# Local-and-summary attention and two MLPs: softmax kept in the PSUM bank of its scores, three units normalised by one instruction

## The reference, cut to what matters

```python
scores_l = scale * q @ k.T                       # masked to |i - j| < 16
scores_s = scale * q @ k_sum.T + log(32)         # k_sum: max over blocks of 32 keys
scores_all = concat([where(mask_l, scores_l, -1e9), scores_s])
a = exp(scores_all - max(scores_all))
a = a / (sum(a) + 1e-9)
x = a @ concat([v, v_sum])                       # v_sum: mean over blocks of 32 values
...
h = x @ w_in;  g = max(h, 0) + alpha * min(h, 0);  x = g @ w_out        # first MLP, 2048 wide
h = x @ w_in2; g = P(h) / (Q(h) + 1e-6);          out = g @ w_out2      # second MLP, rational activation
```

## Time and profile before

| | us |
|---|---|
| median of 3 runs | 654.24 |
| lowest and highest | 653.11 and 656.0 |
| span of the profiled execution, first to last instruction | 652.5 |
| PE busy | 619.4 (95%) |
| DVE busy | 487.2 (75%) |
| ACT busy | 345.9 (53%) |
| POOL busy | 208.5 (32%) |

### The profile page before, as it was taken

The page is one execution under the profiler, slowest core; times in us unless marked ns, Lnnn a source line. Parts: engine busy times, 40 slices in busy tenths (PEclk is TensorE's granted clock), DMA queues, the critical chain, the costliest instruction groups (busy, mean ns, idle before and its releaser), DMA issues.

```text
span 652.5 us, 9963 instructions
## 1 busy us (share of the span) xinstructions
PE 619.4 (95%) x3504; PEld 586.2 (90%) x3504; DVE 487.2 (75%) x1056; ACT 345.9 (53%) x838; POOL 208.5 (32%) x217
## 2 busy tenths in 40 slices
PE   5777899999999999999999997899999999999997
PEld 4767899999999999999999996899999999999995
DVE  3877767555666556555555589999999999999995
ACT  4686544343343353342333275666765576567654
POOL 4545984000000000000122356455443334444431
PEclk9898989999999999999999999999999999999999
DMA  8879920221022201200344410000100010001001
GB/s 183 191 186 244 260 59 14 60 60 41 21 60 48 48 17 33 48 1 4 94 130 130 129 33 1 1 2 0 49 1 1 2 49 0 2 1 49 1 1 49
DMA packets 82211, 37.56 MB, mean 58 GB/s; under 512 B 59761, under 2 KB 76145, under 8 KB 81777
## 3 DMA queue, kind: packets, MB, share of 16 engines
q1 hardware_dynamic: 82160, 36.92, 22.2%
HBM read 32.58 MB, written 3.15 MB: 55 GB/s over the span
## 4 chain that ended last, share of the span: by engine, by line
PE 82%; DVE 11%; ACT 2%; issue 1%; ACTq 0%; DVEq 0%
PE acc L852 12%; PE acc L854 12%; PE acc L853 12%; PE hid L852 9%; PE hid L854 9%; PE hid L853 9%; PE att L852 3%; PE att L854 3%; PE att L853 3%; PE att L841 3%; DVE probs L677 2%; PE att L820 2%; PE att L788 1%; PE att L827 1%; DVE poly L767 1%; DVE g_lo L739 1%
## 5 line engine op out<-in xcount | busy, mean ns | idle before, releaser
L852 PE MATMUL hid<-x_hi,w_in_hi 128*128 128x384 f32 x384 | 130.5, 340 | 0.6 <-DVE x_lo L684 0.6
L854 PE MATMUL hid<-x_hi,w_in_lo 128*128 128x384 f32 x384 | 129.6, 338 | 0.0
L853 PE MATMUL hid<-x_lo,w_in_hi 128*128 128x384 f32 x384 | 129.4, 337 | 0.0
L428 POOL TENSOR_TENSOR w_out_lo<-w_out_raw,w_out_hi 128x512 fp32r<-128x512 f32 x32 | 42.8, 1337 | 246.8 <-ACT w_out_hi L456 246.8
L446 POOL TENSOR_SCALAR qpart<-habs,ab 128x384 f32<-128x384 f32 x64 | 52.3, 817 | 137.8 <-ACT poly L601 136.6
L852 PE MATMUL acc<-g_hi,w_out_hi 128*128 128x384 f32 x256 | 90.9, 355 | 0.0
L853 PE MATMUL acc<-g_lo,w_out_hi 128*128 128x384 f32 x256 | 87.0, 340 | 0.0
L854 PE MATMUL acc<-g_hi,w_out_lo 128*128 128x384 f32 x256 | 87.0, 340 | 0.0
L700 DVE TENSOR_TENSOR g_lo<-g_full,g_hi 128x384 fp32r<-128x384 f32 x64 | 41.2, 644 | 55.3 <-ACT g_hi L456 55.1
L852 PE MATMUL acc<-w_out_hi,g_hi 128*128 128x512 f32 x192 | 76.1, 396 | 5.7 <-DVE g_lo L739 5.7
L854 PE MATMUL acc<-w_out_hi,g_lo 128*128 128x512 f32 x192 | 76.1, 396 | 0.0
(11 more groups left out here) (119 smaller groups left out, 1262.0 us busy)
## 6 DMA issues: line engine op xcount, KB each, us to landing
w_in_raw<-in_moe_w_in_dram SPq DMA_DIRECT2D x32, 256.0 KB, 4.1
w_out_raw<-in_moe_w_out_dram SPq DMA_DIRECT2D x16, 512.0 KB, 4.1
vw<-in_v_dram SPq DMA_DIRECT2D x32, 120.0 KB, 2.6
q_raw<-in_q_dram SPq DMA_DIRECT2D x32, 96.0 KB, 2.6
vs_raw<-in_v_dram SPq DMA_DIRECT2D x4, 768.0 KB, 7.4
out_dram<-out_sb SPq DMA_DIRECT2D x12, 256.0 KB, 2.0
k_raw<-in_k_dram SPq DMA_DIRECT2D x16, 104.0 KB
k_raw<-in_k_dram SPq DMA_DIRECT2D x16, 100.0 KB
```

Source lines behind the costliest of these rows:

```text
L428: pool.tensor_tensor(w_out_lo[:, f, :], w_out_raw[:, f, :], w_out_hi[f][:, :].bitcast(F32), ALU.subtract).then_inc(pool_w_out, 1)
L852: pe.matmul(dst, lhs[0], rhs[0], start=start, stop=False)
L853: pe.matmul(dst, lhs[0], rhs[1], start=False, stop=False)
L854: return pe.matmul(dst, lhs[1], rhs[0], start=False, stop=stop)
```

## The change

The scores stay in the PSUM bank in which PE made them. DVE's masking instruction writes them back to the same columns of `bk[g]`, ACT's exponential works there in place, and its row sums go to three columns at the end of the same bank (columns 384 to 386). `psums` in SBUF goes. `pden` is computed from those columns. The normalisation of a group is one `tensor_tensor` in place of three `tensor_scalar`: it multiplies the 3 x 120 exponentials in PSUM by the three reciprocals, broadcast along the columns from SBUF, and writes `probs` in SBUF. PE's transposes read `probs` as before. No wait is added, removed or moved; the number of ACT and PE instructions stays.

```diff
+        def scores_of(bk, g, u):
+            u -= g * GU
+            return bk[g][:, u * KU:(u + 1) * KU]
+
+        def sums_of(bk, g):
+
+            return bk[g][:, GU * P:GU * P + GU]
...
-                            last = act.activation(probs[:, s, u, :], probs[:, s, u, :], ACT.Exp, scale=-1.0,
-                                                  bias=nmax[:, s, u:u + 1], accum_out=psums[:, s, u:u + 1])
+                            last = act.activation(scores_of(bk, g, u), scores_of(bk, g, u), ACT.Exp, scale=-1.0,
+                                                  bias=nmax[:, s, u:u + 1], accum_out=sums_of(bk, g)[:, u - g * GU:u - g * GU + 1])
...
-                            last = dve.tensor_tensor_reduce(probs[:, s, u, :], bk[g][:, (u - g * GU) * KU:(u - g * GU + 1) * KU],
+                            last = dve.tensor_tensor_reduce(scores_of(bk, g, u), scores_of(bk, g, u),
                                                             mask[:, unit_mask(j, u), :], -1.0 / SQRT_D, 3.0e38,
                                                             ALU.add, ALU.min, nmax[:, s, u:u + 1])
...
-                        dve.tensor_scalar(pden[:, s, us], psums[:, s, us], 1.0e-9, None, ALU.add).then_inc(dve_den, 1)
+                        dve.tensor_scalar(pden[:, s, us], sums_of(bk, g), 1.0e-9, None, ALU.add).then_inc(dve_den, 1)
...
-                        for u in range(g * GU, (g + 1) * GU):
-                            last = dve.tensor_scalar(probs[:, s, u, :], probs[:, s, u, :], prec[:, s, u:u + 1], None, ALU.mult)
-                        last.then_inc(dve_p, 1)
+                        dve.tensor_tensor(probs[:, s, us, :], bk[g][:, 0:GU * KU].rearrange("p (u k) -> p u k", u=GU),
+                                          prec[:, s, us].unsqueeze(2).broadcast_to([P, GU, KU]), ALU.mult).then_inc(dve_p, 1)
```

More of the change, by code:

```diff
@@ L129, in attention_two_mlps @@
     nmax = place("nmax", [P, 2, UNITS])
-    psums = place("psums", [P, 2, UNITS])
     pden = place("pden", [P, 2, UNITS])
```

## The result

| | before | changed kernel |
|---|---|---|
| median, us | 653.67 | 648.54 |
| lowest and highest, us | 652.9 to 656.0 | 648.21 to 649.69 |
| ratio to before, 95% interval | 1 | 0.9908 [0.9886, 0.993] |
| span of the profiled execution, us | 652.5 | 646.4 |

The forecast was 647.0 us with a range of 643 to 651. The changed kernel is 0.9% faster than the one before by the recorded ratio (0.8% by the two medians), and 1.5 us short of the forecast. The forecast took 7.2 us off a median of 654.24. Against the 653.67 us measured beside it the changed kernel gains 5.1 us, and its profiled span is 6.1 us shorter. Its profiled execution took 648.21 us for a span of 646.4, so the distance between the two is 1.8 us, where the forecast had 1.7.

The account below looks back on a forecast made before the run. PE is fully busy from 115 to 300 us; only its earlier stalls, with DVE held by POOL, can go. 0.3 + 4.0 + 1.6 + 1.3 = 7.2 us off 654.24 gives 647.0 us, range 643 to 651.

Parts of the forecast that it names:

- fifth term: From TR of job 6 to the end of the span: forecast 0 us, since everything there shifts as a whole.
- What is held, and by what: Ahead of 115 us: POOL holds DVE instructions with all sources in SBUF, by up to 1.1 us each.
- broadcast operand in SBUF is held all the same: Normalisation: the broadcast reciprocals make the multiplication wait for POOL, one hold a group; 4.2 us gained, 650.0 us, chance 0.13.
- The multiplication: Normalisation of a group: one instruction of 529 ns in place of three taking 0.67 us, 0.14 us shorter undisturbed.
- `pden`, masking, exponentials: Attention chain: `pden` 169 ns undisturbed, masking change taken as 0 within 0.1 us, six exponentials together 0.2 us shorter.
- PSUM instructions are late in every job: Jobs 7 to 15: over 0.08 us more per instruction stalls PE; 661 us at 0.25 us each, chance 0.05.
- Step 4, the landing: Job 5's queries: they land at 65.7 us and hold PE, idle about 3.8 us, limiting the gain to 1.9 us.
- this landing does not move: Job 5's queries: nothing ahead of their issue in SP's queue waits for the attention, so they land at 65.7 us.
- Step 4, the clock: Behind PE's wait for job 5's queries: the clock falls once more, costing 1.6 us.
- no fall of the clock: Behind the DMA wait for job 5's queries: clock stays up; 8.8 us less, 645.4 us, chance 0.15.
- Step 6 and step 10: TR of job 5 gains 4.0 us, the clock behind it 1.6, TR of job 6 1.3; POOL's wait isn't reached.
- What comes later shifts as a whole: After TR of job 6: PE is never idle to 300 us, so the rest moves earlier unchanged.

## Experiments: what held DVE

The theory is that an instruction of DVE is held by POOL when all its sources are in SBUF. Its rival is that fewer instructions do it, wherever their sources are. A further doubt was whether POOL is what holds them. Four kernels part these. The first keeps PSUM and gives back the three instructions:

```diff
-                        dve.tensor_tensor(probs[:, s, us, :], bk[g][:, 0:GU * KU].rearrange("p (u k) -> p u k", u=GU),
-                                          prec[:, s, us].unsqueeze(2).broadcast_to([P, GU, KU]), ALU.mult).then_inc(dve_p, 1)
+                        for u in range(g * GU, (g + 1) * GU):
+                            last = dve.tensor_scalar(probs[:, s, u, :], scores_of(bk, g, u), prec[:, s, u:u + 1], None, ALU.mult)
+                        last.then_inc(dve_p, 1)
```

> The changed kernel with the normalisation of a group cut back into three tensor_scalar instructions, each reading its 120 exponentials from PSUM. If the gain comes from where the source lies (theory): each multiplication stays at 0.25 to 0.32 us with POOL busy, none is held, TR of jobs 5 and 6 has no idle time, and the time is that of the changed kernel, 648.5 us, up to 1 us more. If it comes from one instruction in place of three, so that DVE meets POOL less often (rival): multiplications of up to 1.3 us are back, with 2 to 4 us of idle time of PE in TR of jobs 4 to 6, and the time is 651 to 653 us.

It took 647.25 us, ratio 0.9906 [0.9884, 0.9928], the time of the changed kernel within the intervals (the expectation had 648.5 and up). The line view of 10 to 115 us, where POOL works, has 24 of the 42 instructions in this row; the 18 in the other banks are at 334 to 344 ns:

```profile
L684 DVE TENSOR_SCALAR probs<-att,prec x24: 332/334/344, 14.2 to 95.9; 128x120 f32<-128x120 f32 x24
```

None is held. Each takes 334 ns, though, where the same instruction took 276 ns from SBUF: from PSUM it is 58 ns longer, and above the 0.25 to 0.32 us that was expected. PE still waits 0.77 and 0.62 us in TR of job 4, so a short wait there is no sign of a hold. In TR of jobs 5 and 6 it doesn't wait.

The second is the kernel before with the one instruction, and both sources in SBUF:

```diff
-                        for u in range(g * GU, (g + 1) * GU):
-                            last = dve.tensor_scalar(probs[:, s, u, :], probs[:, s, u, :], prec[:, s, u:u + 1], None, ALU.mult)
-                        last.then_inc(dve_p, 1)
+                        dve.tensor_tensor(probs[:, s, us, :], probs[:, s, us, :],
+                                          prec[:, s, us].unsqueeze(2).broadcast_to([P, GU, KU]), ALU.mult).then_inc(dve_p, 1)
```

> The kernel before, its scores, exponentials and sums in SBUF, with only the three multiplications of a group made one tensor_tensor, both sources in SBUF. Theory (the place of the source): the one instruction is held by POOL and ranges from 0.53 to 1.7 us, pden from 0.15 to 1.3 us, PE is idle for 0.5 to 2 us in TR of job 5; 650 to 652 us. Rival (fewer instructions are what counts): it stays under 0.8 us nearly always and the time is 648 to 649.5 us, that of the changed kernel.

It took 647.39 us, ratio 0.9902 [0.9882, 0.9922]. The lines in 10 to 115 us, then PE's timeline at TR of jobs 4 and 5:

```profile
L676 DVE TENSOR_TENSOR probs<-probs,prec x14: 532/533/1462, 14.1 to 99.6; 128x360 f32<-128x360 f32 x14
...
L672 DVE TENSOR_SCALAR pden<-psums x14: 157/170/2055, 13.7 to 99.2; 128x3 f32<-128x3 f32 x14
```

```profile
55.14 0.85 PE L826 MATMUL att<-ident,probs 128*120 128x128 f32 x3 [2.21 <-DVE probs L676]
...
80.25 0.54 PE L826 MATMUL att<-ident,probs 128*120 128x128 f32 x3 [2.19 <-DVE probs L676]
```

Here DVE is held as before, up to 1462 and 2055 ns, but once for the multiplication of a group in place of up to three times. PE still stands 2.2 us in TR of job 4 and of job 5, and not at all in TR of job 6. At 647.39 us both expected ranges were missed (650 to 652 and 648 to 649.5). The kernel is as fast as the changed one by its median and not by the same way. PE comes to job 5's keys late enough (65.78 us) not to wait for the DMA, so it loses no clock there, and it doesn't have the loss of the fifth term (its period of four steps, explained below, is 20.73 us). So equal times say nothing here on the theory; the rows do. They show that the source decides on the hold, and the number of instructions on how often it is paid.

The third is the changed kernel with the row sums back in SBUF, so that `pden` alone reads SBUF. `psums` is again where it was:

```diff
+    psums = place("psums", [P, 2, UNITS])
...
-                                                  bias=nmax[:, s, u:u + 1], accum_out=sums_of(bk, g)[:, u - g * GU:u - g * GU + 1])
+                                                  bias=nmax[:, s, u:u + 1], accum_out=psums[:, s, u:u + 1])
...
-                        dve.tensor_scalar(pden[:, s, us], sums_of(bk, g), 1.0e-9, None, ALU.add).then_inc(dve_den, 1)
+                        dve.tensor_scalar(pden[:, s, us], psums[:, s, us], 1.0e-9, None, ALU.add).then_inc(dve_den, 1)
```

> The changed kernel with the row sums back in SBUF (psums), so that pden has its source in SBUF and is the only instruction of the chain that POOL can hold. Theory: pden ranges from 0.15 to 1.3 us while POOL splits weights and stays at 0.17 us without POOL; job 5's chain has about 0.9 us to spare in the changed kernel, so at most one such hold is covered and PE is idle for 0 to 1.5 us in TR of jobs 5 and 6; 648.5 to 650.5 us. Rival (the part of pden is nothing): 648.5 us and no idle time.

Groups by line (busy us, mean ns of one) in 10 to 115 us, and PE's timeline at TR of job 4:

```profile
L680 DVE TENSOR_SCALAR pden<-psums 128x3 f32<-128x3 f32 x14 | 6.7, 482 | 1.9 <-ACT att L496 1.0 <-ACT acc L496 0.6
...
L684 DVE TENSOR_TENSOR probs<-att,prec 128x360 f32<-128x360 f32 x8 | 4.3, 533 | 0.3
```

```profile
51.70 0.54 PE L834 MATMUL att<-ident,probs 128*120 128x128 f32 x3 [0.47 <-DVE probs L684]
53.34 0.55 PE L834 MATMUL att<-ident,probs 128*120 128x128 f32 x3 [1.10 <-DVE probs L684]
```

The multiplication is free at 533 ns and `pden`, three columns, is held to 482 ns on average. That costs 1.57 us ahead of TR of job 4, where PE would have waited for the DMA anyway, and nothing in job 5. The time is 644.95 us, ratio 0.9861 [0.9842, 0.9881]: faster than the changed kernel by 3.6 us of medians, and under the 648.5 us from which both expectations started, although it does strictly worse on DVE. Of the 3.4 us between the two profiled spans, 1.6 lie behind TR of job 6: this was the first sign that the place of the tiles matters. Another 1.2 us lie behind job 5's queries, where the clock did not fall in this execution (11.12 us to TR of job 5 for 12.32).

The fourth leaves DVE as it was before and takes POOL's work away (what it leaves out is said in its expectation):

```diff
-                pool.tensor_tensor(w_in_lo[:, f, :, :], w_in_raw[:, f, :, :], w_in_hi[f][:, :, :].bitcast(F32),
+                pool.tensor_tensor(w_in_lo[:, f, 0, 0:16], w_in_raw[:, f, 0, 0:16], w_in_hi[f][:, 0, 0:16].bitcast(F32),
...
-                pool.tensor_tensor(w_out_lo[:, f, :], w_out_raw[:, f, :], w_out_hi[f][:, :].bitcast(F32),
+                n = DM if m else 16
+                pool.tensor_tensor(w_out_lo[:, f, 0:n], w_out_raw[:, f, 0:n], w_out_hi[f][:, 0:n].bitcast(F32),
```

> The kernel before with POOL's splits of the first MLP's weights cut from 512 to 16 columns; the products of the first MLP take the high part of the weights in place of the low one, so their matmuls have the same number and shapes. It leaves out the low parts of the first MLP's weights. Theory (POOL holds DVE): with scores in SBUF as before, the multiplications are all at 0.27 to 0.29 us but where POOL sums blocks of values, PE has no idle time in TR of jobs 4 to 6, it waits for job 5's keys and queries at about 65.7 us, and the time is 646 to 649.5 us. Rival (something else slows DVE in this stretch, such as the DMAs into SBUF): multiplications of up to 1.3 us stay and the time is 652 to 654 us.

```profile
L678 DVE TENSOR_SCALAR probs<-probs,prec 128x120 f32<-128x120 f32 x42 | 12.1, 344 | 0.5
...
L701 DVE TENSOR_TENSOR g_lo<-g_full,g_hi 128x384 fp32r<-128x384 f32 x13 | 7.4, 569 | 19.8 <-ACT g_hi L457 19.8
```

In 10 to 115 us the multiplication from SBUF is down to 344 ns on average, from 594 in the kernel before, and `g_lo` to 569 ns from 808, with no edit of DVE's program. Not all holds are gone: the longest multiplication still takes 1152 ns. What is left shows the cause best. POOL's sums of value blocks were not cut, and the groups of three multiplications that are still held fall into the time of these sums. First POOL, then DVE:

```profile
19.23 5.49 POOL L413 TENSOR_TENSOR vs_raw<-vs_raw 96x1024 f32<-96x1024 f32 x5 [0.21 <-DMA vs_raw<-in_v_dram]
```

```profile
22.00 1.87 DVE L678 TENSOR_SCALAR probs<-probs,prec 128x120 f32<-128x120 f32 x3
...
27.81 0.67 DVE L678 TENSOR_SCALAR probs<-probs,prec 128x120 f32<-128x120 f32 x3
```

Up to 25 us, while POOL sums, groups take 0.79 to 2.01 us, and from 27.81 us on each takes 0.66 or 0.67. PE waits 0.45 and 0.44 us in TR of job 4, and not in TR of jobs 5 and 6. The time is 644.76 us, ratio 0.9862 [0.9841, 0.9883], below the expected 646 to 649.5. The rows show POOL's instructions to be the cause of the holds.

## Experiments: where 1.56 us went

The period of four steps, from one job's keys to the next, is a clean gauge, since PE is never idle from 115 to 300 us. It is read from PE's timeline at the keys of the jobs. In the kernel before:

```profile
241.70 0.51 PE L788 MATMUL att<-ident,k_raw 100*128 100x100 f32 x4
...
262.44 0.51 PE L788 MATMUL att<-ident,k_raw 100*128 100x100 f32 x4
```

and in the changed one:

```profile
234.82 0.51 PE L794 MATMUL att<-ident,k_raw 100*128 100x100 f32 x4
255.71 0.51 PE L794 MATMUL att<-ident,k_raw 100*128 100x100 f32 x4
```

That is 20.74 against 20.89 us for the same matmuls, at full clock and without idle time. Jobs with four tiles of 104 keys have 21.13 and 21.22. The removal of `psums` moves `pden`, `prec`, `g_full`, `g1_hi` and `g1_lo` down by 64 bytes. The last three, which are the large ones, began 32 bytes behind a multiple of 128 and now begin 96 behind one. Two kernels test this from both sides. One gives the changed kernel its 64 bytes back and leaves them free:

```diff
+    top += 64
     pden = place("pden", [P, 2, UNITS])
```

> The changed kernel with 64 bytes left free where psums stood, so that pden, prec, g_full, g1_hi and g1_lo are at the offsets of the kernel before (the change had moved them 64 bytes down). From job 7's TR to the end of the span the kernel before and the run with its sums in SBUF take 525.3 us, the changed kernel 526.7 us, at no idle time that differs. Theory (the offset of the tiles sets PE's pace): a period of four steps falls from 20.89 to 20.73 us, the stretch to 525.3 us, the time is 1.4 us under the changed kernel's 648.5: 647.1 us, or 645 us where the clock does not fall. Rival (row sums in PSUM slow PE): no change, 648.5 us and 20.89 us.

The other moves the tiles of the kernel before, whose instructions stay all the same:

```diff
-    psums = place("psums", [P, 2, UNITS])
     pden = place("pden", [P, 2, UNITS])
     prec = place("prec", [P, 2, UNITS])
     g_full = place("g_full", [P, CH])
     g1_hi = place("g1_hi", [P, R1, CH], F32R)
     g1_lo = place("g1_lo", [P, R1, CH], F32R)
+    psums = place("psums", [P, 2, UNITS])
```

> The kernel before with psums placed behind the other tiles of this part of SBUF, so that pden, prec, g_full, g1_hi and g1_lo move 64 bytes down as in the changed kernel; nothing else. Theory (offset): a period of four steps goes from 20.73 to 20.89 us and the time is 1.4 us longer than the kernel before, a ratio of 1.002. Rival: no difference, ratio 1.000 and 20.73 us.

The same rows of PE's timeline, for the padded kernel and for the one before with its tiles moved:

```profile
234.27 0.51 PE L795 MATMUL att<-ident,k_raw 100*128 100x100 f32 x4
255.00 0.51 PE L795 MATMUL att<-ident,k_raw 100*128 100x100 f32 x4
```

```profile
241.76 0.51 PE L788 MATMUL att<-ident,k_raw 100*128 100x100 f32 x4
262.64 0.51 PE L788 MATMUL att<-ident,k_raw 100*128 100x100 f32 x4
```

The period is 20.73 and 20.88 us: it goes with the place of the tiles, in either program, and not with PSUM. The padded kernel took 645.48 us, ratio 0.9858 [0.9833, 0.9883], 3.1 us under the changed kernel by medians. Only 1.5 us of that can be put down to the tiles; the rest is ahead of 115 us, where executions differ (below, step 4). The kernel before with its tiles moved took 655.18 us, ratio 1.0006 [0.999, 1.0022]. By its time alone no loss is shown, and the expected 1.4 us (0.21%) is just inside the interval; what shows it is the period.

A third place asks what it is about the place:

```diff
+    top += 32
     pden = place("pden", [P, 2, UNITS])
```

> The changed kernel with 32 bytes left free where `psums` was, in place of 64. `g_full`, `g1_hi` and `g1_lo` then begin at 0 modulo 128 bytes; in the kernel before and in the one padded by 64 bytes they begin at 32, in the changed kernel at 96. The period of four steps without idle time was 20.73 us at 32 and 20.89 us at 96, in each of two kernels. Theory (a start in the second half of 128 bytes is what costs): the period is 20.73 us, the span some 1.3 us under the changed kernel's at like idle times. Rival (the place of 32 is special, or the distance to the other tiles matters and not the place in 128 bytes): 20.8 us or more.

```profile
233.01 0.51 PE L795 MATMUL att<-ident,k_raw 100*128 100x100 f32 x4
253.80 0.51 PE L795 MATMUL att<-ident,k_raw 100*128 100x100 f32 x4
```

20.79 us, between the two (one execution: 645.61 us, span 643.8). The theory of the second half (20.73) falls. The rival had 20.8 or more, and is just about met (the other periods of this kind are at 20.79 and 20.80), but it names no cause: the three places give 20.73, 20.79 and 20.89 us at 32, 0 and 96 bytes. Which of the five moved tiles does it, and why, is left open. The extra time isn't only in the matmuls that read `g1_hi` and `g1_lo`. The products of `hid`, whose operands did not move, are longer too; their group in 115 to 245 us, first for the changed kernel, then for the padded one (2 ns each, which is little beside the period's 0.15 us, and the half-padded kernel has 338 as well):

```profile
L858 PE MATMUL hid<-x_hi,w_in_hi 128*128 128x384 f32 x100 | 34.0, 340 | 0.0
```

```profile
L859 PE MATMUL hid<-x_hi,w_in_hi 128*128 128x384 f32 x100 | 33.8, 338 | 0.0
```

During these DVE and ACT write and read the moved tiles, so it may be their traffic that disturbs PE's reads. That is an argument and not a measurement.

## Experiments: what caps the gain

The forecast let the landing of job 5's queries hold PE. To test it, these loads go ahead of two weights and of the block values, in the changed kernel and in the one before:

```diff
+            load_keys(5)
             load_w(0, 4)
             load_v_blocks(2)
-            load_keys(5)
```

> The changed kernel with load_keys(5) issued ahead of load_w(0, 4) and load_v_blocks(2), so that job 5's keys and queries land some 4 us earlier and the weights and blocks behind them some 2 us later. Theory (the landing holds PE in step 4, and the clock falls behind the wait): PE has no idle time ahead of job 5's transposes, which start at about 62.6 in place of 64.9 us, the clock does not fall there, and the next bound is POOL's w_in_lo of step 6 at about 72.6 us; 645.5 to 647 us. Rival (the gain has been taken in full and the landing holds nothing): 648.5 us.

> The kernel before with the same move of load_keys(5). Theory: there PE comes to job 5's transposes 1.9 us after the queries have landed, so their landing earlier is worth nothing: ratio 0.999 to 1.001, PE at job 5's keys at 67.2 us as before. Rival (the order of the DMAs is worth the same in both kernels): ratio 0.996.

In the changed kernel PE came to the keys without idle time at 62.47 us, 2.4 us earlier than 64.91. Nothing was won: 649.04 us, ratio 0.9915 [0.9894, 0.9936], against an expected 645.5 to 647. PE's timeline at step 6, and POOL's ahead of it, show the next wait:

```profile
73.80 0.44 PE L858 MATMUL hid<-x_hi,w_in_hi 128*128 128x384 f32 x1 [2.81 <-POOL w_in_lo L430]
```

```profile
66.40 5.67 POOL L420 TENSOR_TENSOR vs_raw<-vs_raw 96x1024 f32<-96x1024 f32 x5 [6.37 <-DMA vs_raw<-in_v_dram]
72.16 0.24 POOL L424 TENSOR_SCALAR vsum<-vs_raw 96x64 f32<-96x64 f32 x1
72.48 1.27 POOL L430 TENSOR_TENSOR w_in_lo<-w_in_raw,w_in_hi 128x512 fp32r<-128x512 f32 x1
```

The block values now land later, POOL idles 6.37 us for them with the weights of step 6 queued behind, and PE waits 2.81 us for these. This is the wait that the forecast had looked at and found "not reached": PE would come at 73.6 us, POOL be done at 71.0. It was right, with a margin of 2.6 us, and in the changed kernel the margin was 4.0 (POOL done at 70.77, PE there at 74.78 us). The move of the loads used that up. In the kernel before, PE doesn't wait for these keys, and the same move won nothing: 656.64 us, ratio 1.0032 [1.0017, 1.0047]. It is even 2.2 us slower, outside the expected 0.999 to 1.001, and why is open. Its trace shows 14.47 us from TR of job 4 to job 5's keys, where the kernel before has 14.46, so nothing is lost there; of the 3.2 us that its span is longer, 2.6 are there before TR of job 4 (55.41 for 52.79 us), ahead of the place where the moved loads are issued.

The last run takes the block values out of the way too and pads the tiles:

```diff
+    top += 64
...
-            load_w(0, 4)
-            load_v_blocks(2)
             load_keys(5)
+            load_w(0, 4)
             load_w(0, 5)
             load_w(0, 6)
             load_values(5)
+            load_v_blocks(2)
             load_w(0, 7)
-            load_v_blocks(3)
             for j in range(NPAIR + 2, JOBS):
                 load_keys(j)
                 load_values(j)
+                if j == NPAIR + 2:
+                    load_v_blocks(3)
...
-                if f in (5, 11):
-                    summarise_values(2 + f // 8)
+                if f in (8, 12):
+                    summarise_values(2 + f // 12)
```

> The changed kernel with 64 bytes left free where `psums` was, the keys and queries of job 5 loaded ahead of two weights and of the block values, as in the run with the keys early, and the block values of chunks 1 and 2 loaded and summed later (POOL sums them in steps 8 and 12 in place of 5 and 11), so that POOL has nothing between the keys' arrival and the low weights of step 6. The whole computation is done. With the keys early alone, PE came to step 6 at 71.0 us and stood 2.81 us for POOL, whose sum of block values took 66.4 to 72.1 us. Theory (that sum is what took the gain away, and the 64 bytes are worth 1.4 us): no idle time of over 0.5 us from 62 us on; TR of job 5 at 77.04 - 2.81 = 74.2 us in place of 77.92; the period of four steps behind 115 us 20.73 us; the median 644 to 642 us, 2 to 3 us under that of the padded kernel (645.48). Rival (the weights of step 6 themselves are late, since two of their loads now stand behind the keys): PE stands at step 6 for 1 to 3 us all the same, with ACT's rounding or a DMA as releaser, and the median is 645 to 646 us, no better than the padded kernel's.

It took 641.01 us (640.49 to 641.56), ratio 0.9811 [0.9784, 0.9839], 7.5 us under the changed kernel, 12.4 under the one before as measured beside it, and 4.5 under the padded kernel, where 2 to 3 were expected. Short waits of 0.46 and 0.30 us stay in TR of job 4. From 57 us on PE is at full clock and not idle; two stretches, and TR of job 5:

```profile
57.00:67.60 10.60, 10.60 (x67) 10.56 (x67) 7.36 (x12) 7.06 (x16) 9.67 (x8) 1.00 1.10 318
64.00:68.00 4.00, 4.00 (x27) 4.00 (x26) 3.93 (x5) 1.30 (x3) 2.67 (x3) 1.00 1.19 282
```

```profile
73.04 0.82 PE L835 MATMUL att<-ident,probs 128*120 128x128 f32 x6
```

TR of job 5 is at 73.04 us, 4.9 us ahead of the changed kernel's (1.0 us of this was there in TR of job 4 already), where 74.2 was expected; the period is 20.73 us. So the cap was the order of the loads in SP's queue, as the step on the landing had it, together with the order of POOL's work, which takes over once the first is changed.

## Experiment: the cost of a PSUM destination

```diff
-                            last = act.activation(scores_of(bk, g, u), scores_of(bk, g, u), ACT.Exp, scale=-1.0,
+                            last = act.activation(scores_of(bk, g, u), probs[:, s, u, :], ACT.Exp, scale=-1.0,
...
-                            last = dve.tensor_tensor_reduce(scores_of(bk, g, u), scores_of(bk, g, u),
+                            last = dve.tensor_tensor_reduce(probs[:, s, u, :], scores_of(bk, g, u),
```

> The changed kernel, but the masking instruction writes its scores to `probs` in SBUF, as before the change, and the exponential reads them there and writes to the PSUM bank. All of the computation is done. In the kernel before (SBUF to SBUF) one exponential began 0.382 us after the other, in the changed kernel (PSUM to PSUM) 0.295 us; the masking took 279 ns with the result in SBUF and 323 ns in PSUM. Theory A (the destination makes the exponential faster): spacing 0.30 to 0.33 us. Theory B (the source does, since ACT at 384 columns took 491 ns from PSUM and 526 ns from SBUF): spacing 0.35 to 0.38 us. By either the masking is back at 279 ns, which shows that the 44 ns are those of the destination. The span changes by less than 1 us, since jobs 7 to 15 hide both.

First the masking of the changed kernel (min/median/max ns), then that of this one:

```profile
L671 DVE DVE_READ_ACCUMULATOR2_ANT nmax<- x96: 83/141/146, 12.1 to 284.8; 128x1 f32 x96
L671 DVE CUSTOM_DVE_ANT_0 att<-att,mask x78: 280/323/327, 11.9 to 284.6; 128x120 f32<-128x120 f32 x78
```

```profile
L671 DVE DVE_READ_ACCUMULATOR2_ANT nmax<- x96: 81/83/85, 12.4 to 281.1; 128x1 f32 x96
L671 DVE CUSTOM_DVE_ANT_0 probs<-att,mask x78: 273/279/283, 12.2 to 280.9; 128x120 f32<-128x120 f32 x78
```

The destination in PSUM costs DVE 44 ns in the instruction and 58 ns in the accumulator read behind it. The exponentials of one job, in ACT's timeline, are in the changed kernel

```profile
115.84 0.34 ACT L495 ACTIVATE att<-att,nmax 128x120 f32<-128x120 f32 x1 [4.16 <-DVE nmax L671]
...
117.33 0.41 ACT L495 ACTIVATE att<-att,nmax 128x120 f32<-128x120 f32 x1
```

and with the source in SBUF

```profile
112.54 0.36 ACT L495 ACTIVATE att<-probs,nmax 128x120 f32<-128x120 f32 x1
...
113.89 0.39 ACT L495 ACTIVATE att<-probs,nmax 128x120 f32<-128x120 f32 x1
```

From PSUM to PSUM it is five steps in 1.49 us, 0.298 us each. From SBUF to PSUM it is four steps in 1.35 us, 0.338 us each (a first step of 0.44 us stands ahead of them), and the kernel before, from SBUF to SBUF, was at 0.382. So the source gives 0.040 us, in the direction of theory B. The other 0.044 us are not shown to be the destination's, as theory A had it: against the kernel before, this one has the row sums in PSUM too. The kernel with its sums in SBUF, whose exponentials go from PSUM to PSUM, tells the two apart:

```profile
114.27 0.33 ACT L496 ACTIVATE att<-att,nmax 128x120 f32<-128x120 f32 x1
...
115.62 0.35 ACT L496 ACTIVATE att<-att,nmax 128x120 f32<-128x120 f32 x1
```

That is four steps in 1.35 us, 0.338 us each, where the changed kernel has 0.298. The two differ in the place of the sums, and by 64 bytes in the place of some tiles. That this second difference plays no part is seen in the padded kernel, with its sums in PSUM and its tiles where the kernel with sums in SBUF has them: its steps are 0.29 to 0.31 us. The sums give 0.040 us, the source 0.040, and if the parts add up, the destination of the exponentials gives next to nothing. ScalarE: Activation LUTs in the Trainium skill, section "Step-by-step: what each stage is for", calls PSUM the faster destination of ACT. No run here shows it for the 120 columns; the row sums, which ACT writes too, agree with 0.040 us.

This kernel's one execution took 644.58 us; since it is one, and since its keys of job 5 came early (62.48 us), nothing more is read from that time.

## Why the prediction was right, point by point

*What is held, and by what.* Right. With the source in PSUM no instruction is held; with most of POOL's work gone, those from SBUF are at 344 ns on average in place of 594, and those still held stand beside the POOL work that was left. The rival that the broadcast operand in SBUF is held all the same is refuted by 531/532/534 ns. It had priced one hold a group at 650.0 us; the kernel that has this, with both sources in SBUF, took 647.4, since it avoids the DMA wait and the slow clock that I had counted for it.

*The multiplication.* 529 ns forecast, 532 measured. On the Trainium skill's rule (VectorE: DVE Perf Modes, "Why PSUM operands drop a tier") the runs give both answers. The `tensor_scalar` went from 276 to 334 ns with its source in PSUM, 58 ns for 120 columns and 0.17 us for a group, beside the estimated 0.19 us from that page. The `tensor_tensor` took 532 ns with its large source in either memory. The rule agrees where there is one tensor source, and it says nothing against the form that the change uses.

*`pden`, masking, exponentials.* `pden` took 161 ns for 169. The masking was taken at 0 with bounds of 0.1 us; it is 0.04 us longer by the spacing (0.24 for 0.20 us), within them. The exponentials were taken 0.035 us shorter each, by their source, and are 0.085 us shorter: 0.040 by the source and 0.040 by the place of the sums, which the forecast had taken at 0. Six of each together are 0.3 us shorter, which PE doesn't see after job 6. The rival in which PSUM instructions are late in every job (from 0.08 us more each) thus never began.

*Step 4, the landing.* Right in kind: a DMA ends the wait, at 64.91 us for the keys, and the queries follow at 65.60, forecast 65.7. Two sizes were off. PE was idle 2.18 us there and not 3.8, for it came to the keys 4.5 us earlier than before and not 5.7. 0.30 us of the stall stayed, and the jobs ahead ran 0.4 us late in this execution. The other 0.5 us lie in the stretch whose lower clock was priced at 1.6 us: it took 10.60 us before (56.65 to 67.25 us) and 9.53 now (53.20 to 62.73), 1.07 less; the kernel with its keys early took 9.10. PE would only have waited the longer for the same landing, and so this cost nothing. And "this landing does not move" holds for the cause but not for the number. In the kernel of the last experiment, whose loads are in the same order, the view of the queries' issues reads

```profile
L255 SPq DMA_DIRECT2D q_raw<-in_q_dram x2: 483/1173/1863, 54.4 to 56.3; - x2
```

where the changed kernel has 56.5 to 58.6 and the kernel before 56.0 to 57.6. PE then began the queries at 63.09 us. Over the seven kernels with this order of loads in which PE waited for them, it began the queries between 63.09 and 65.64 us. The jobs ahead shift too (job 4's second transposes at 50.31 us in that execution and 53.20 in the changed kernel), and what moves both is open. That 65.7 was hit to 0.1 us is therefore luck in part.

*Step 4, the clock.* Right in the profiled execution: 0.59 from 64 to 68 us, at a cost of 1.06 us for 1.6. But the argument for it, the length of the wait, does not hold, and it was close to the other case. Over the kernels the waits of PE for job 5's keys and queries were 3.05, 2.18, 2.05 and 1.89 us where the clock fell behind them (POOL shortened, changed, half padding, padding), and 1.82, 1.69 and 1.52 us where it did not (sums in SBUF, three instructions, exponential from SBUF). The rival "no fall of the clock" described those. This looks like a limit between the two lists, but longer waits elsewhere were followed by full clock. PE waited 2.81 us for POOL in the kernel with its keys early, and 2.19 us in TR of job 5 in the kernel with one instruction from SBUF; the stretches behind them:

```profile
75.00:80.00 5.00, 5.00 (x32) 4.96 (x31) 1.66 (x4) 2.32 (x5) 5.00 (x4) 1.00 1.05 279
```

```profile
80.00:84.00 4.00, 3.75 (x24) 3.75 (x25) 3.28 (x5) 2.06 (x4) 4.00 (x3) 1.00 1.04 168
```

In that second kernel the 2.21 us in TR of job 4 did bring the clock down (0.50 from 56 to 58 us), and in the kernel before the 2.63 us ahead of job 3's transposes did not (1.00 from 41 to 48 us). The forecast of a fall was thus right partly by luck: the length of a wait alone does not decide, and what does is open.

*Step 6 and step 10.* 3.85 and 2.87 us for 4.0 and 2.9. The wait for POOL in step 6 was rightly found not to be reached.

*After that.* "What comes later shifts as a whole" is the step that failed. I had looked at the tiles' contents and not at their addresses: taking 64 bytes out of the middle of the layout made PE 0.09 to 0.16 us slower in each period of four steps, which is nearly all of the 1.56 us. With the 64 bytes left in, the profiled span is 645.0 us, where the forecast had 645.3; that execution was the slowest of four (646.84 us, median 645.48), so the closeness is luck in part as well.

## What to carry to other kernels

Where DVE is late only while POOL is at work, compare the maximum of each of DVE's lines with its median: what was held here is the instruction with all its sources in SBUF, and a source in PSUM freed it. Where a stall is taken away, follow the queue to the next thing that lands or is computed late, here a DMA and behind it POOL, since the gain ends there until that order is changed too. And when a change removes or adds a tile, keep the addresses of the others, or measure a kernel that only moves them.

## What was not expected of the hardware

- The same matmuls of PE, at full clock without idle time, take 20.73, 20.79 or 20.89 us a period with three tiles beginning 32, 0 or 96 bytes behind a multiple of 128.
- ACT's exponential of 120 columns with its row sum starts every 0.382 us with all in SBUF, every 0.338 with either the source or the sum in SBUF and the rest in PSUM, and every 0.298 with all in PSUM.
- DVE's masking instruction takes 279 ns with its result in SBUF and 323 ns in PSUM, and the accumulator read behind it 83 and 141 ns; a `tensor_scalar` of 120 columns takes 276 ns from SBUF and 334 from PSUM, while a `tensor_tensor` of 360 takes 532 ns from either.
- A DMA wait of 1.89 us (in two parts, 1.74 and 0.15) was followed by the lower clock, while waits of 2.19, 2.63 and 2.81 us elsewhere were not.
